# ScalarE's high part of the gates' product in front of y's copies in the third step, and the first half of the next K*R product with it

## What is computed

```python
for t in range(S):                       # B=4, H=8, S=768, D=48
    cur = einsum('bhd,bhe->bhde', u * k[t], v[t])
    y[t] = einsum('bhd,bhde->bhe', r[t], state + cur)
    state = w[t][..., None] * state + einsum('bhd,bhe->bhde', k[t], v[t])
x = y as (3072, 384)
x = ((x @ w1) * (x @ w2) @ w3) @ w_out   # 384 -> 1024 -> 1024 -> 384
P = exp(x @ w_gate), scaled 8 times by rows and columns   # 3072 x 8
out = sum over e of P[:, e] * (relu(x @ w1[e]) @ w2[e])
```

## Time and profile before

| | |
|---|---|
| timed runs | 2094.85, 2099.29, 2099.54 us; median 2099.29 us |
| the profiled execution | 2097.74 us, its span 2095.7 us |
| granted TensorE clock, mean | 0.995 |
| TensorE busy (PE) | 2024.5 us, 97% |
| VectorE busy (DVE) | 1230.6 us, 59% |
| ScalarE busy (ACT) | 802.0 us, 38% |
| GpSimd busy (POOL) | 770.5 us, 37% |
| chain that ended last | PE 55%, issue 25%, DVE 8%, POOL 5%, DMA 3%, ACT 3% |
| units 2 to 10 | 128 to 475 us, one every 40 us |

### The profile page before, as it was taken

How to read it: one execution, slowest core, us unless ns; L and a number is a source line. 1 busy time by engine, 2 the same in 40 slices (tenths; PEclk the granted TensorE clock), 3 DMA queues, 4 the chain that set the end, 5 groups by cost and what they waited for, 6 DMA issues and landing times.

```text
span 2095.7 us, 40062 instructions
## 1 busy us (share of the span) xinstructions
PE 2024.5 (97%) x16048; PEld 1679.1 (80%) x16048; DVE 1230.6 (59%) x1891; ACT 802.0 (38%) x1448; POOL 770.5 (37%) x1011
## 2 busy tenths in 40 slices
PE   7899999999999989999999999999999999999998
PEld 4699999899877768778778888788877888878877
DVE  3677777774686665656664554554465554455454
ACT  4555555554433333333343333333343333333332
POOL 2375775771476576664240111110142110111111
PEclk9999999999999999999999999999999999999999
DMA  8443343331266667665444454434443444443432
GB/s 207 94 121 111 101 123 112 96 106 29 76 229 225 245 207 256 233 231 197 164 136 156 138 174 142 145 131 164 139 155 113 150 138 173 139 156 131 162 130 101
DMA packets 118584, 316.10 MB, mean 151 GB/s; under 512 B 11920, under 2 KB 45616, under 8 KB 118400
## 3 DMA queue, kind: packets, MB, share of 16 engines
q1 hardware_dynamic: 102768, 259.38, 38.4%
q0 software_dynamic: 14944, 53.68, 7.4%
q10 hardware_dynamic: 688, 0.48, 0.1%
HBM read 239.87 MB, written 71.27 MB: 148 GB/s over the span
## 4 chain that ended last, share of the span: by engine, by line
PE 55%; issue 25%; DVE 8%; POOL 5%; DMA 3%; ACT 3%; SPq 0%; POOLq 0%; ACTq 0%; DVEq 0%
PE ps L1502 13%; PE ps L1504 13%; PE ps L1503 13%; PE ps L1306 3%; PE ps L1307 3%; PE ps L1308 3%; POOL x L716 2%; PE ps L1329 2%; PE ps L1379 2%; DVE h_lo L1239 1%; DVE R L1082 1%; PE ps L1418 1%; DMA w_rows<-batch 1%; DVE xs_lo L1047 1%; DMA w_raw<-w 1%
## 5 line engine op out<-in xcount | busy, mean ns | idle before, releaser
L716 POOL TENSOR_TENSOR x<-x,tmp 128x512 f32<-128x512 f32 x126 | 168.0, 1359 | 803.4 <-DVE tmp L1252 802.1
L1504 PE MATMUL ps<-h_hi,w 128*128 128x512 f32 x1152 | 456.1, 396 | 0.0
L1502 PE MATMUL ps<-h_hi,w 128*128 128x512 f32 x1152 | 455.3, 395 | 0.0
L1503 PE MATMUL ps<-h_lo,w 128*128 128x512 f32 x1152 | 455.0, 395 | 0.0
L794 ACT ACTIVATE tb<-ps 128x512 f32<-128x512 f32 x378 | 226.4, 599 | 515.3 <-PE ps L1504 495.4
L983 ACT ACTIVATE h_hi<-tb 128x512 fp32r<-128x512 f32 x378 | 238.7, 632 | 458.7 <-DVE tb L1234 246.7
L1230 DVE TENSOR_TENSOR tb<-tb,ps 128x512 f32<-128x512 f32 x252 | 172.2, 685 | 289.6 <-PE ps L1504 284.3
L1239 DVE SCALAR_TENSOR_TENSOR h_lo<-tb,h_hi 128x512 fp32r<-128x512 f32 x378 | 306.0, 811 | 41.4 <-ACT h_hi L983 35.6
L1234 DVE TENSOR_TENSOR tb<-ps,tb 128x512 f32<-128x512 f32 x252 | 173.8, 691 | 233.6 <-PE ps L1504 232.5
L1503 PEld LDWEIGHTS ps<-h_lo,w 128*128 128x128 f32 x1152 | 218.0, 189 | 51.5
L1502 PEld LDWEIGHTS ps<-h_hi,w 128*128 128x128 f32 x1152 | 217.1, 188 | 50.7
(11 more groups left out here) (155 smaller groups left out, 3258.5 us busy)
## 6 DMA issues: line engine op xcount, KB each, us to landing
early<-w_rows SPq DMA_DIRECT2D x63, 1024.0 KB, 5.5
late<-w_rows SPq DMA_DIRECT2D x63, 896.0 KB, 5.2
w<-w_rows SPq DMA_DIRECT2D x128, 384.0 KB, 4.3
w_rows<-batch POOLq DMA_DIRECT2D x105, 384.0 KB, 3.6
w_rows<-w SPq DMA_DIRECT2D x64, 384.0 KB, 2.6
Pb<-p_rows SPq DMA_DIRECT2D x24, 512.0 KB, 6.2
w_raw<-w POOLq DMA_DIRECT2D x16, 576.0 KB, 6.1
w_raw<-w SPq DMA_DIRECT2D x16, 576.0 KB, 5.0
```

The lines of the kernel that those rows point to most:

```text
L716: return gp.tensor_tensor(to, a, b, ALU.add)
L1502: mm(o, w_hi, x_hi, start=start, stop=False, skip_group_check=True)
L1503: mm(o, w_hi, x_lo, start=False, stop=False, skip_group_check=True)
L1504: return mm(o, w_lo, x_hi, start=False, stop=stop, skip_group_check=True)
```

## The change

In step 3 of units 1 to 12 ScalarE makes the high part of the gates' product, where there is one, before it copies y, and not after. VectorE makes the first half of the next unit's K*R at the end of step 3, no longer of step 4; the second half stays at the end of step 5. No instruction is added or removed.

```diff
@@ -930,6 +930,8 @@
                     if k == 0:
                         copy_keys(u - 1)
                     if k == 3:
+                        if n >= 0:
+                            take_ab(n)
                         copy_last_y(u - 1)
                         copy_y(u - 1)
                 if u < U:
@@ -938,7 +940,8 @@
                     if k == 7:
                         copy_at64(u)
                 if n >= 0:
-                    take_ab(n)
+                    if not (1 <= u <= U and k == 3):
+                        take_ab(n)
                     if n and n % NF == 0:
                         copy_x2(n // NF - 1)
                     if n - 1 in GATE_AT:
@@ -1176,8 +1179,8 @@
                     split_ab(n)
                 if 1 <= u <= U and k == 4:
                     take_x(u - 1)
-                if u + 1 < U and k in (4, 5):
-                    make_ruk(u + 1, k - 4)
+                if u + 1 < U and k in (3, 5):
+                    make_ruk(u + 1, k // 5)
                 if s >= SLICES + 7:
                     i = 2 * (s - SLICES - 7)
                     for p in X_FIRST[i:i + 2]:
```

## The result

| | before | after |
|---|---|---|
| timed runs | 5: 2094.85 to 2099.54 us | 5: 2083.51 to 2087.44 us |
| median | 2095.09 us | 2086.66 us |
| ratio | | 0.9949, interval 0.9934 to 0.9963 |
| profiled execution, its span | 2097.74, 2095.7 us | 2086.66, 2084.7 us |
| PE, DVE, ACT, POOL busy | 2024.5, 1230.6, 802.0, 770.5 us | 2022.2, 1228.6, 801.2, 773.9 us |

Faster, by 8.4 us in the medians and 10.7 us by the ratio. The median of before is of five runs here; the three shown ahead of the prediction had 2099.29. Lines behind the edits have numbers higher by 3 in the changed kernel (by 1 or 4 where an experiment adds one): 1344, 1376 and 1382 are 1341, 1373 and 1379 of before.

The account below looks back on a forecast made before the run. TensorE, busy 97% of the span, was taken as the bound: 6.7 us from nine units plus 0.6 from unit 1 made 7.3 us, 2090.4 us from the profiled execution, forecast 2091 us; range 2085 to 2098 us.

Parts of the forecast that it names:

- What bounds the kernel: TensorE, busy 97% of the span; only its waits at lines 1373 and 1379 can be won, 1.54 us a unit.
- Part one: Units 2 to 12, step 3: ScalarE's high part of the gates' product before y's copies; 0.14 us a unit by itself.
- Part two: Units 0 to 10: first half of K*R moves from step 4 to 3, hidden only behind part one; 0.60 us.
- Nine units, 6.7 us: Units 2 to 10: both parts together save 0.74 us a unit of TensorE's waiting, 6.7 us in all.
- Unit 1, 0.6 us: Unit 1 has no gates, but its step 6 waits 1.89 us for VectorE with K*R's first half on that path.
- Rival A: Step 3: moved K*R meets GpSimd's Rpad copy and ends late; a unit keeps 0.21 us, 2096 us; chance 0.10.
- the margin of 0.7 us: Unit 6, step 3: K*R's first half ends at 278.8, 0.7 us before GpSimd's copies start at 279.51.
- the quoted rule: Two-input VectorE and SBUF-reading GpSimd instructions exclude each other for a whole instruction; order of issue decides who blocks.
- B: Second stage: gain given back, as GpSimd's batches and stores keep their own time; about 2098 us; chance 0.13.
- C: Levels' whole 0.47 us passes and later work partly escapes GpSimd's block copies; up to 1.15 us a unit, 2087 us; chance 0.11.
- D: Step 3: ScalarE waits for a late gates' product before copying y; 6 us and more slower, 2105 us; chance 0.05.
- the two frames: Profiled execution of 2097.74 us and three timed runs of 2094.85 to 2099.54 us; forecast put between them at 2091 us.

Follow-up runs that it names:

- both halves in step 3: Changed kernel with the second half of K*R also moved to step 3, behind the first; ratios 0.9953 and 0.9946 against the kernel before, medians 2084.19 and 2081.99 us.
- the control: The kernel before measured again with no edit, as if it were a change; ratio 0.9996 (0.9985 to 1.0007), nine units 358.62 us.
- part one alone: Kernel before with only ScalarE's high part moved in front of y's copies, K*R left in steps 4 and 5; ratio 0.9983, nine units 357.12 us.
- the first trace: First profiled execution of the kernel before, no edit, from which the prediction's rows were read; 2097.74 us.

## Why the prediction was right and wrong

**What bounds the kernel: right.** TensorE's waits at lines 1373 and 1379 were the whole of what could be won in the units: with both halves in step 3 they are gone but for one of 0.2 us, and TensorE is busy for all but 0.4 us of nine units.

**Part one, 0.14 us a unit: right.** 0.17 alone. The step that carried it was the reading of unit 11, where the next limit is seen (the gates' copy waits for TensorE), in place of taking the level's 0.47 us for the gain.

**Part two, 0.60 us, hidden only behind part one: right.** 0.00 alone, 0.60 on top of part one.

**Nine units, 6.7 us: right to 0.3 us**; 7.0 us measured. At the last score of unit 6, 0.68 us are lost, where the prediction had 0.80. Unit 1, 0.6 us: its wait in step 6 went from 1.89 to 1.29 us in all three traces of the changed kernel, and is 1.89 in the control and with part one alone:

```profile
84.24 0.76 PE L1376 MATMUL ps<-Rpad,K 128*32 128x32 f32 x64 [1.29 <-DVE K L1087]
```

**Rival A** didn't come about in the nine units: K*R is the first of the two in each, and GpSimd's copies take 2.13 us as before. But the margin of 0.7 us was read from an unusual unit; what kept the rival away is the order, the prediction's other reason. In unit 6 GpSimd starts 0.07 us before K*R ends. This is not the change's doing: from the end of the gates' product to y's second copy the first trace has 2.21 us in unit 6 (277.21 to 279.42), because y came 0.6 us later there and the gates' product 0.3 us earlier, and the control, the same kernel, has the 1.35 us of the changed one (272.03 to 273.38):

```profile
273.87 0.42 DVE L1132 TENSOR_TENSOR ab<-ps,ab 128x256 f32<-128x256 f32 x1 [0.61 <-ACT ab L794]
275.64 0.81 ACT L794 ACTIVATE x<-ps 128x768 fp32r<-128x768 f32 x1 [1.36 <-PE ps L1420]
```

Units 3, 4, 7, 9 and 10 of the first trace have 1.3 to 1.6 us already. So in six of the nine units K*R ends between 0.2 us before and 0.1 us after the start of GpSimd's copies, and only in units 2, 5 and 8 is the margin 0.7 us or more. In unit 1 the two do meet, K*R first by 0.02 us: GpSimd's copies take 3.00 us in place of 2.48 and the first operation of the level 1.52 in place of 1.00, which the wait in step 6 doesn't feel, as the prediction had it. Both halves together meet GpSimd in unit 6 too, and as the quoted rule of the Trainium skill (SBUF — State Buffer, section "Who interferes with whom") has it, the order decided: GpSimd was the one that waited, 0.54 us. **B** is not shown; the mean of the three ratios (8.4 us) leaves nothing to give back from 7.6. **C and D** didn't come about.

**Where it was wrong: from the sum to the predicted time.** The sum said 7.3 us less, and the median of before turned out to be 2095.09 us (2094.12 and 2094.26 in the later medians of 26 and 17 runs), so that 2095.1 - 7.3 = 2087.8 us would have stood against the 2086.66 measured. I wrote 2091, "between the two frames", which against 2095.09 is a change of 4.1 us where 8.4 were measured. The step that failed is the one that read the profiled execution (2097.74) and the median of three runs (2099.29) as frames of the kernel; they lay 2.6 and 4.2 us above that median. They are draws: the profiled execution carried 1.7 us of TensorE at its lower clock in step 3 of unit 1, 0.6 us in unit 6 and a second stage 3.2 us longer than the control's, where TensorE was busy 4.0 us longer, in part at its lower clock. The same draw makes 11.0 us of the first pair of profiles where the change is worth 7.6. And the range, 2085 to 2098 us, was laid around that frame: it held the time only in its lowest fifth.

The term that was mis-sized is what differs from execution to execution outside the nine units. In eleven traces of seven kernels unit 2 began between 95.0 and 99.5 us, and the second stage took 1526.6 (part one alone) to 1543.4 us (both halves), 1533.3 us for the same kernel the next time. I had given it 2 us. Of the second stage's length, TensorE's busy time is 1496.5 to 1502.9 us, for the same instructions, and its idle time 30.1 to 40.9 us. One wait, some 220 us into the stage, is 4.7 to 10.3 us of that; what makes it long or short was not followed up.

## What to carry to other kernels

Where one unit of work has no such operation or no such neighbour (here unit 11), it shows in the old trace where the chain will be cut off after the change; subtract it from a normal unit rather than adding up durations. Two moves can be worth 0.2 and 0.0 apart and 0.8 together, when the first opens the idle time in which the second hides, so look at the idle time's position in the engine's order, not only at its length. For changes of a few tenths of a per cent, read the repeated part of the trace unit by unit, where it repeats to 0.1 us, and take the whole run's median and the one profiled execution for draws with several us of their own. Before a margin is read from one unit, compare that unit's length and its waits with those of the others: unit 6 was 0.6 us longer than its own repeat, and its margin of 0.7 us was not there in the next trace.

## What the runs showed of the hardware

TensorE ran the same ten products in 3.49 us in some executions and in 5.18 or 6.20 us in others of the same program, after idle times of 2.7 to 3.0 us, with mean granted clocks of 1.00 and 0.79 in the window around the ten of 3.49 and of 5.18 us. A VectorE operation with two inputs in SBUF lengthened GpSimd's two copies from 2.13 to 2.67 us when it was first, and itself took 1.22 us in place of 0.42 when it was second. In the place beside GpSimd's block copies a half of K*R and a scaling of R of the same size took 1.10 us each, against 0.68 elsewhere.
